# A channel network computed as seven half-sized products, in two phases over three groups of tokens

## What is computed

```python
attn = softmax(mask(q k^T / 8 + slope * -|i - j|)) v      # window of 128 keys, 4 x 8 heads, 576 positions, 64 wide
x = attn as (4, 576, 512)
u = x + ((x^T U) V)^T                                     # U: 576 x 32, V: 32 x 576
y = u + relu(u @ w_ch1) @ w_ch2                           # 512 -> 2048 -> 512: the channel network
h = relu(y @ w_in); a, b = halves of h                    # 512 -> 1024
b = (b - mean(b)) / sqrt(var(b) + 1e-6)
out = (a * (w_spatial @ b + b_spatial)) @ w_out           # 576 x 576 along the positions, then 512 -> 512
```

## Time and profile before

| | us |
|---|---|
| runs: median (lowest to highest) | 774.51 (774.31 to 775.64) |
| profiled execution | 774.84 |
| its span, first to last instruction | 773.1 |
| TensorE busy | 758.4 |
| VectorE / ScalarE / GpSimd busy | 288.1 / 265.2 / 111.3 |
| HBM read / written | 27.83 MB / 4.72 MB |

### The profile page before, as it was taken

One profiled execution on the slowest core, in us unless ns is written; L12 is line 12 of the kernel. 1 busy time (PEld: TensorE's weight loads), 2 busy tenths in 40 slices (PEclk: granted clock), 3 DMA queues, 4 the chain that ended last, 5 costly groups with the idle time before them and its releaser, 6 DMA issues.

```text
span 773.1 us, 12362 instructions
## 1 busy us (share of the span) xinstructions
PE 758.4 (98%) x4584; PEld 647.9 (84%) x4584; DVE 288.1 (37%) x807; ACT 265.2 (34%) x670; POOL 111.3 (14%) x95
## 2 busy tenths in 40 slices
PE   6999999799999999999999999999999999999998
PEld 4777777578888998888888888888899899998998
DVE  6878777531112113111311113111547417435431
ACT  5877777532322112111210102123343243342422
POOL 1212113344451000000000000123410010100100
PEclk9999999999999999999999999999999999999999
DMA  6333331213322000000000000012100010100101
GB/s 170 111 93 122 93 97 60 82 58 106 109 82 69 1 1 1 1 2 0 1 0 0 0 0 0 27 42 74 56 1 1 20 43 0 46 15 0 61 1 62
DMA packets 24692, 33.04 MB, mean 43 GB/s; under 512 B 2768, under 2 KB 11984, under 8 KB 24656
## 3 DMA queue, kind: packets, MB, share of 16 engines
q1 hardware_dynamic: 24656, 32.56, 13.2%
HBM read 27.83 MB, written 4.72 MB: 42 GB/s over the span
## 4 chain that ended last, share of the span: by engine, by line
PE 96%; DVE 1%; issue 1%; DMA 0%; ACT 0%; POOL 0%; SPq 0%; POOLq 0%; DVEq 0%; ACTq 0%
PE bank L1153 9%; PE bank L1154 9%; PE bank L1152 8%; PE bank L1166 6%; PE bank L1167 6%; PE bank L1168 6%; PE bank L1020 4%; PE wide L1035 3%; PE bank L1002 2%; PE bank L1268 2%; PE bank L1270 2%; PE bank L1269 2%; PE bank L1141 2%; PE bank L1139 2%; PE wide L1167 2%; PE wide L1166 2%
## 5 line engine op out<-in xcount | busy, mean ns | idle before, releaser
L834 DVE SCALAR_TENSOR_TENSOR rl<-bank,rh 128x512 fp32r<-128x512 f32 (+1 forms) x80 | 51.0, 638 | 308.3 <-ACT rh L558 308.3
L558 ACT ACTIVATE rh<-bank 128x512 fp32r<-128x512 f32 (+1 forms) x80 | 44.4, 555 | 312.0 <-PE bank L1154 312.0
L1152 PE MATMUL bank<-uh,w1h 128*128 128x512 f32 (+1 forms) x320 | 118.0, 369 | 0.0
L1153 PE MATMUL bank<-uh,w1l 128*128 128x512 f32 (+1 forms) x320 | 117.9, 368 | 0.0
L1154 PE MATMUL bank<-ul,w1h 128*128 128x512 f32 (+1 forms) x320 | 117.9, 368 | 0.0
L1166 PE MATMUL bank<-rh,w2h 128*128 128x512 f32 (+1 forms) x240 | 88.6, 369 | 0.0
L1168 PE MATMUL bank<-rl,w2h 128*128 128x512 f32 (+1 forms) x240 | 88.4, 368 | 0.0
L1167 PE MATMUL bank<-rh,w2l 128*128 128x512 f32 (+1 forms) x240 | 88.4, 368 | 0.0
L467 ACT ACTIVATE sc<-sc,mn 128x256 f32<-128x256 f32 (+1 forms) x144 | 66.9, 468 | 22.0 <-DVE mn L725 22.0
L1152 PEld LDWEIGHTS bank<-uh,w1h 128*128 128x128 f32 x320 | 60.4, 189 | 10.0
L1154 PEld LDWEIGHTS bank<-ul,w1h 128*128 128x128 f32 x320 | 60.4, 189 | 9.9
(11 more groups left out here) (160 smaller groups left out, 1480.4 us busy)
## 6 DMA issues: line engine op xcount, KB each, us to landing
qkraw<-qk SPq DMA_DIRECT2D x32, 288.0 KB, 3.0
out_t<-tok SPq DMA_DIRECT2D x16, 288.0 KB, 2.1
vraw<-v_n SPq DMA_DIRECT2D x16, 256.0 KB, 2.7
w1raw<-w SPq DMA_DIRECT2D x16, 256.0 KB, 2.9
w2raw<-w SPq DMA_DIRECT2D x16, 256.0 KB, 2.6
w1raw<-w_in SPq DMA_DIRECT2D x8, 256.0 KB, 2.8
w1raw<-w_sp SPq DMA_DIRECT2D x4, 288.0 KB, 2.8
w1raw<-w_out SPq DMA_DIRECT2D x4, 256.0 KB, 2.5
```

The costliest lines, as they stand in the source:

```text
L834: dve.scalar_tensor_tensor(out=rl[:, j % 2, 0:width(c)], in0=r_ps[j % 2][:, 0:width(c)], scalar=0.0, in1=rh[:, j % 2, 0:width(c)], op0=ALU ...
L1152: pe.matmul(o, w1h[:, j, k, :], uh[:, k, 0:w], start=(k == 0), stop=False)
L1153: pe.matmul(o, w1l[:, j, k, :], uh[:, k, 0:w], start=False, stop=False)
```

## The change

The product of a 2304 x 512 by a 512 x 2048 matrix, and the one that follows, are both computed with Strassen's scheme in Winograd's form: each operand is cut in 2 x 2 blocks, seven products of half-sized sums replace eight, and the four blocks of the result are sums of the products. The tokens form three groups of 768 (two halves of 384: all channel matmuls have 384 columns).

First phase: 24 units (3 groups x 8 pairs of hidden blocks), each of seven products `up(s, m)` of six matmuls. Some sums of the result are made by letting one product add into the bank of another; for the others ScalarE copies a partial sum out (`keep_p`, after products 1, 6 and 7), and VectorE adds it (`c11`, `c12`, `c22`). ScalarE applies the relu to the sums in place. Each unit's four relu'd blocks (786 KB) are stored to `r_scr` in HBM. The weight sums S1 to S4 are made on VectorE, their high parts on ScalarE, low parts on GpSimd and VectorE: for w1 in the first units, for w2 in units 9 to 14, 17 and 18 (`W2_UNIT`), from where the split w2 goes to `w2_scr` in HBM. `x_sum` (GpSimd) and `x_sum1` (VectorE) make the input sums in place, `hi_xs` and `lo_xs` split them.

Second phase: 168 ring entries (3 groups x 7 products x 8), each of six matmuls in `down(g, m)`. The relu'd blocks come back (`raw` a, b, c, d, over `tok`), GpSimd makes the sums t3, t2, t4 (`r_sum`, two halves of 1536 columns each), VectorE t1 (`r_sum1`); `hi_r` and `lo_r` split one block of 384 columns for each entry into a ring of 5. The split w2 comes back in seven pieces of 2.1 MB (`w2q`). The tensor u was stored to HBM and comes back in `u_in`; GpSimd's `add_res` and VectorE's `dc`, `dc21` add it, and the result goes through HBM (`x2_scr`) to the third stage. That stage's instructions are unchanged; SBUF is laid out anew, its weights come in another order, and its first waits change.

The core of the diff (removed are `up`, `down`, `hi_r`, `lo_r`, `hi_u`, `lo_u`, `keep_x2` and the loads of before):

```diff
+G = 3
+HT = TOK // (2 * G)
+UNITS = NF // 2
+NU = G * UNITS
+RING = 5
+QP = 2 * P
...
+UP = []
+for _s in range(NU):
+    UP += [(_s, 1)] + ([(_s - 1, 4), (_s - 1, 3)] if _s else []) + [(_s, m) for m in (2, 6, 5, 7)]
+UP += [(NU - 1, 4), (NU - 1, 3)]
+UP_AT = {x: n + 1 for n, x in enumerate(UP)}
...
+for _g in range(G):
+    DN += [(_g, 1)] + ([(_g - 1, 3), (_g - 1, 4)] if _g else []) + [(_g, m) for m in (2, 6, 5, 7)]
+DN += [(G - 1, 4), (G - 1, 3)]
+DN_AT = {x: (n + 1) * UNITS for n, x in enumerate(DN)}
+ENTRY = {x: n * UNITS for n, x in enumerate(DN)}
+ENTRIES = [(g, m, kk) for g, m in DN for kk in range(UNITS)]
+W2_UNIT = {9: 0, 10: 1, 11: 2, 12: 3, 13: 4, 14: 5, 17: 6, 18: 7}
...
+LATE = 19
...
+            def load_w1(u):
+                if u >= 2:
+                    sp.wait_ge(w1_low, 2 * (u - 1))
+                    sp.wait_ge(w1_sum, 4 * (u - 1))
+                for i, j in ((0, u), (1, u + UNITS)):
+                    slot = (2 * u + i) % 4
+                    sp.dma_start(w1raw[:, slot, 0:DM], w1[j]).then_inc(w1_in[slot], 16)
+            def store_u(g, r):
+                sp.wait_ge(u_kept, u_ready(g, r))
+                t = slice(2 * g * HT, 2 * (g + 1) * HT)
+                sp.dma_start(u_scr[2 * r:2 * r + 2, :, t].rearrange("k p t -> p k t"),
+                             tok[:, 2 * r:2 * r + 2, t]).then_inc(u_out[r], 16)
+            def store_r(s):
+                g, u = divmod(s, UNITS)
+                sp.wait_ge(r_relu, 3 * (s + 1))
+                sp.wait_ge(c21_done, s + 1)
+                sp.dma_start(r_scr[g, u], r_stage(s)).then_inc(r_out[s % 2], 16)
+            def load_w2(kk):
+                if kk == 0:
+                    sp.wait_ge(w1_low, 2 * UNITS)
+                    sp.wait_ge(w1_sum, 4 * UNITS)
+                else:
+                    sp.wait_ge(w2_low, 2 * kk)
+                    sp.wait_ge(w2_sum, 4 * kk)
+                for i, j in ((0, kk), (1, kk + UNITS)):
+                    sp.dma_start(w1raw[:, i, 0:DM], w2[j * P:(j + 1) * P, :]).then_inc(w1_in[i], 16)
+            def store_w2(kk):
+                sp.wait_ge(w2_slow, kk + 1)
+                sp.wait_ge(w2_low, 2 * (kk + 1))
+                for h, parts in ((0, w2_top), (1, w2_bot)):
+                    sp.dma_start(w2_scr[A11, :, h, kk, :], parts[0]).then_inc(w2_out, 16)
+                    q = parts[1] if h == 0 else parts[1].rearrange("p (q c) -> p q c", c=QP)
+                    sp.dma_start(w2_scr[A12:A22 + 1, :, h, kk, :].rearrange("q p c -> p q c"),
+                                 q).then_inc(w2_out, 16)
+                    sp.dma_start(w2_scr[S1:S4 + 1, :, h, kk, :].rearrange("q p c -> p q c"),
+                                 parts[2]).then_inc(w2_out, 16)
+            def load_w2q(m):
...
+            for s in range(NU):
+                if s + 2 < UNITS:
+                    load_w1(s + 2)
+                if s == 2:
+                    store_u(2, 0)
+                    store_u(2, 1)
+                if s >= 1:
+                    store_r(s - 1)
+                if s in W2_UNIT:
+                    store_w2(W2_UNIT[s])
+                if s + 1 in W2_UNIT:
+                    load_w2(W2_UNIT[s + 1])
+                if s == LATE + 1:
+                    sp.wait_ge(w2_out, 6 * 16 * UNITS)
...
+            sp.wait_ge(up_p, UP_AT[(NU - 2, 3)])
+            load_w2q(5)
+            sp.wait_ge(up_p, UP_AT[(NU - 1, 3)])
+            load_raw(0, "c", 0)
+            load_raw(0, "c", 1)
+            store_r(NU - 1)
+            load_w2q(7)
+            load_w2q(4)
+            sp.wait_ge(u_out[0], 16 * G)
+            sp.wait_ge(u_out[1], 16 * G)
+            sp.wait_ge(c11_done, NU)
+            sp.wait_ge(c12_done, NU)
+            sp.wait_ge(c22_done, NU)
+            load_u(0, 11)
+            load_u(0, 12)
+            for i in range(2):
+                sp.wait_ge(r_out[i], 16 * NU // 2)
+            load_w2q(3)
+            load_u(0, 22)
+            store_x2(0, 11)
...
+            next_raw(1, "a", 1)
...
+            def r_sum(g, m, h):
+                u = slice(4 * h, 4 * h + 4)
+                a, b, c, d = (raw[n][:, u, :] for n in "abcd")
+                if m == 3:
+                    pool.wait_ge(raw_in["b"][h], 16 * (g + 1))
+                    pool.wait_ge(raw_in["c"][h], 16 * (g + 1))
+                    pool.tensor_tensor(b, c, b, ALU.subtract).then_inc(rt3, 1)
+                elif m == 2:
+                    pool.wait_ge(rt3, 2 * g + h + 1)
+                    pool.wait_ge(rk_lo, ENTRY[(g, 1)] + 4 * h + 4)
+                    pool.tensor_tensor(a, a, b, ALU.add).then_inc(rt2, 1)
+                else:
+                    pool.wait_ge(rt2, 2 * g + h + 1)
+                    pool.wait_ge(rk_lo, ENTRY[(g, 2)] + 4 * h + 4)
+                    pool.tensor_tensor(d, d, a, ALU.subtract).then_inc(rt4, 1)
+            def add_res(g, n):
+                kept, done, i = {11: (dp1_kept, dp1_u, 0), 12: (du2_kept, du2_u, 1), 22: (du3_kept, du3_u, 2)}[n]
+                pool.wait_ge(u_back[0 if n in (11, 22) else 1], 32 * g + (16 if n != 22 else 32))
+                for m in range(2):
+                    pool.wait_ge(kept, 2 * g + m + 1)
+                    o = sums_d[:, i, m]
+                    pool.tensor_tensor(o, o, u_in[:, 0 if n in (11, 22) else 1, m], ALU.add).then_inc(done, 1)
...
+            for s in range(NU):
+                g, u = divmod(s, UNITS)
...
+                if s + 2 < UNITS:
+                    w1_low_of(s + 2)
+                if s in W2_UNIT:
+                    w2_low_of(W2_UNIT[s])
+                if u == UNITS - 1 and g < G - 1:
+                    x_sum(g + 1, 4)
+            for g in range(G):
+                add_res(g, 11)
+                for m in (3, 2, 4):
+                    r_sum(g, m, 0)
+                    r_sum(g, m, 1)
+                if g == G - 1:
+                    for m in range(WU):
+                        lo_wc(m)
...
+            def w2_hi_of(kk):
+                act.wait_ge(w2_out, 6 * 16 * kk) if kk else act.wait_ge(xs_lo, 14)
+                for i in range(2):
+                    act.wait_ge(w1_in[i], 16 * (UNITS // 2 + kk + 1))
+                act.activation(w2_top[0].bitcast(F32R), w2_ra[:, 0:QP], ACT.Copy).then_inc(w2_hi, 1)
+                act.activation(w2_top[1].bitcast(F32R), w2_rb.rearrange("p (q c) -> p q c", c=QP),
...
+            def keep_p(s, m):
+                i, kept, freed = {1: (0, p1_kept, c11_done), 6: (1, u2_kept, c12_done),
+                                  7: (2, u3_kept, c22_done)}[m]
+                act.wait_ge(up_p, UP_AT[(s, m)])
+                if s:
+                    act.wait_ge(freed, s)
+                act.activation(sums_u[:, i, :], a_ps[s % 2][:, 0:HT], ACT.Copy).then_inc(kept, 1)
...
+            def hi_r(n):
+                g, m, kk = ENTRIES[n]
+                if n >= RING:
+                    act.wait_ge(rk_used, n - RING + 1)
+                if kk % 4 == 0:
+                    h = kk // 4
+                    if m <= 3:
+                        act.wait_ge(raw_in[RAW_OF[m]][h], 16 * (g + 1))
+                    else:
+                        act.wait_ge({4: rt4, 5: rt1, 6: rt2, 7: rt3}[m], 2 * g + h + 1)
+                act.activation(rk[:, n % RING, 0], raw[RAW_OF[m]][:, kk, :], ACT.Copy).then_inc(rk_hi, 1)
+            def keep_dp(g, m):
...
+            step(B - 1, 2)
+            hi_xs(0, 2)
+            hi_xs(0, 6)
+            step(B - 1, 3)
...
+            for s in range(1, NU):
+                g, u = divmod(s, UNITS)
+                keep_p(s, 1)
+                if u == 0:
+                    hi_xs(g, 7)
+                if s == 1:
+                    hi_t(B - 1)
+                if s + 2 < UNITS:
+                    w1_room(s + 2)
+                    w1_hi_of(s + 2)
+                if s in W2_UNIT:
+                    w2_hi_of(W2_UNIT[s])
+                relu(s - 1, 3)
+                c21(s - 1)
...
+                relu(s - 1, 1)
+                keep_p(s, 6)
...
+                if s + 2 < UNITS:
+                    w1_shi_of(s + 2)
+                if s in W2_UNIT:
+                    w2_shi_of(W2_UNIT[s])
+                relu(s, 0)
+                keep_p(s, 7)
...
+            def room(s):
+                if s >= 2:
+                    dve.wait_ge(r_out[s % 2], 16 * (s // 2))
+            def c11(s):
+                dve.wait_ge(up_p, UP_AT[(s, 2)])
+                dve.wait_ge(p1_kept, s + 1)
+                if s == 0:
+                    dve.wait_ge(xs_lo, 7)
+                    dve.wait_ge(u_out[0], 16)
+                    dve.wait_ge(u_out[1], 16)
+                room(s)
+                dve.tensor_tensor(r_stage(s, 0), e_ps[:, 0:HT], sums_u[:, 0, :], ALU.add).then_inc(c11_done, 1)
...
+            def lo_r(n):
+                g, m, kk = ENTRIES[n]
+                dve.wait_ge(rk_hi, n + 1)
+                dve.tensor_tensor(rk[:, n % RING, 1], raw[RAW_OF[m]][:, kk, :], rk[:, n % RING, 0],
```

(39 more changed lines are left out.)

976 lines of the change are left out of this document (680 added, 296 removed).

## The result

The changed kernel takes 903.2 us (median of 4 runs, 901.4 to 905.7), the kernel before, measured with it, 774.7 (774.3 to 775.6): ratio 1.166, 95% interval 1.164 to 1.168. It is slower by 128 us. The forecast was 890, with a range of 828 to 935. The profiled execution has a span of 903.9 us against 773.1.

What follows compares the result with a forecast made beforehand. The prediction took TensorE's unbroken matmul stream (busy 98% of the span) as the bound. From 774.84 us it took off a 45.2 gain and added 161 of waits: 890.6, stated as 890, range 828 to 935.

Steps and rivals of the forecast that it cites:

- The gain: TensorE's channel matmuls: 395.5 us before, 350.3 us after as 2016 matmuls of 384 columns; 45.2 us saved.
- Rival E: Matmuls of 384 columns come every 0.19 us instead of every 0.174: +32 us; chance 0.02.
- w2 rounds: Units 10 to 14 and 18: chain of stores, load, copies and sums takes 17.2 us against a 7.3 us unit; +58 (48 to 72).
- Rival A: Transfers faster, or loads and stores passing one another: rounds 42, queue 4, first group 28, total 858 us; chance 0.14.
- First group: Start of second phase: GpSimd's add_res waits for u_in, sums stand behind it; +40 us (28 to 48).
- VectorE against GpSimd: Second phase: GpSimd's r_sum steps hold up VectorE's lo_r, both operands in SBUF; +21 us (5 to 34).
- rival B: A long GpSimd step doesn't hold VectorE to its end: 21 falls to 2, first group to 34, total 865; chance 0.11.
- The term of 5: End: hi_wc(8..11) in the middle of the last product and hi_wc(12..16) ahead of relu_v(0); +5 us (1 to 10).
- Start and first units: Start +9 (3 to 14): waits for x sums and lo_xs; first units +12 (5 to 18): longer unit chains, late load_w1(5).
- Queue, group changes, end, clock: DMA queue before second phase +8, first-phase group changes +4, end copies of hi_wc +5, low clock after idle stretches +4 us.
- Rival C: Faster: TensorE isn't held by the w2 rounds, all waits together 42 us, total 771.5 us; chance 0.06.

Runs made afterwards that it cites:

- combined2: Changed kernel with w2 stores in two parts, t3 and t2 on VectorE, t4 of group 0 ahead of add_res, earlier start, c and u_in ahead of w2q(5): 832.6 us.

## Why the prediction was right, and where its terms were off

The forecast is 13 us under the measured 903.2. Two terms were 28 us too small together (groups 1 and 2, and the start with the first units), the third stage 2, and the others some 14 too large together, so part of the closeness is luck: errors of both signs met. The largest terms and their mechanisms held.

**The gain, 45.2 against 46.1.** Right: an entry of six matmuls comes every 1.04 us. Rival E fell: the steps are 0.173 us, though weight loads are listed with 209.

**w2 rounds, 58 against 54.9.** The chain was right link by link, and shown: with its stores divided it loses 22.9. The term was oversized because its data took 8.8 us instead of 9.7. Rival A had the direction right, here and in the queue before the second phase: in the page's two slices from 407 to 452 us, with rows of 16 KB among others, 406 and 416 GB/s were moved, where the forecast had 380, and u_in came at 27.3 instead of 32. It had the size too large both times. The estimate of 7.4 us for a round's data, worked out from the Trainium skill, "DMA: Bandwidth & Descriptors", section "Anatomy of one DMA", which has its fit for another issuing path, is lower than the 8.8 measured with rows of 1 KB. Rival A as a whole, 858, didn't come.

**First group, 40 against 35.8.** Right in mechanism: add_res in GpSimd's order, shown by the run that moves it (14.7 back), and t3 and t2 at 3.4 us each behind it.

**VectorE against GpSimd, 21 against 24.0.** Right, and rival B fell: lo_r stands at 3.82 us beside a step of 3.88, and with the sums cut down group 1 ran without a gap. I had priced it by where the sums stand, 9.5 us at t3 and t2 and 1 at t4, and that is where group 1 lost 9.4 and 1.9. The budget of 62 us in 58.2 says that some 4 us per group stay however the sums are cut; it doesn't give the size.

**The missing term: group 2, 11.0.** The prediction put 5 us on ScalarE's copies of the third stage's weights "in the middle of the last product" and ahead of relu_v. It said nothing of hi_wc(0..7) and hi_x2 among the ring copies of (2, 2) and (2, 4), nor of GpSimd's differences of the same weights beside lo_r, though both stand in the order of the code. The term of 5 itself was too small: 2.5 us of the 11.0 lie in the last product, and the third stage took 7.1 more.

**Start and first units, 21 against 35.2.** The largest error. The stores of u ahead of load_w1(5) were priced as "7.4 us late" within a term of 12, and their move gave back 9.4; units 3 to 7 lost 13.0 in all. Most of the error lies before: the first product came 4.6 us later where the forecast had 2, and from it to unit 3 another 17.6 us were lost, where the forecast had 7 and some 0.9 a unit. The failed step is "half of the first unit behind that: 7": it priced the waits for lo_xs, and neither the w1 sums beside them (5.4 us longer in the trace, though only 2.1 came back when they were moved), nor the waits for ScalarE's copies and VectorE's last tok, nor the slow steps after each wait. How the 17.6 us divide among these isn't settled. The granted clock is 0.91 from 120 to 160 and 0.84 from 160 to 200 us there.

**Queue, group changes, end, clock.** 5.2, 3.9, 7.1 and nothing of its own, against 8, 4, 5 and 4. The clock's share lies in the other terms: up to 0.5 us in a round, and in groups 1 and 2 some 7.8 of the 35.0 us are steps of 0.32 us in place of 0.17, an upper bound, since TensorE would have waited for lo_r in part of that time. Filling the waits raised the mean clock and didn't change the time. At the third stage TensorE waits 4.79 us for ScalarE's vr, which stands behind hi_wc(12..16), as forecast.

**Rival C**, the faster one, didn't come: TensorE was held ahead of product (s, 7) in every round. Other orders didn't reach it either: with all that the runs point to, 823 us remain. By product starts, `combined2` (832.6) still loses some 22 us in rounds, 12 + 5 + 21 in the groups, 19 in units 0 to 7 and 7 in the third stage, and more than the gain of 46 is gone before the rest is counted. I tried no way of making the w2 pieces without the store to memory.

## What to carry to other kernels

A change that takes work from the full engine and gives it to idle ones is worth its gain only if their steps don't form a chain: go through every buffer that is filled, sent away and filled again, and count the time from its last use to its next data against the period in which it is needed. Send each part of such a buffer as soon as it is done, and put nothing that waits for a transfer ahead of work that is ready: these two edits gave back 35 and 12 us here. Where VectorE and GpSimd both take two operands from SBUF, look at what each long step will stand beside, and add their times as if they were one engine for the least that they can cost. Beside a ring of a few entries spread every row of extra copies; that was worth 4 us.

## What the runs showed of the hardware that I had not expected

- The exclusion of VectorE and GpSimd holds both ways and at every length met: 3.82 us listed for a 0.55 us step, 4.95 and 4.86 for 1.76, and GpSimd's 3.4 us step listed with 4.87. The listed start is that of the waiting, so a long listed step isn't slow work. Cutting GpSimd's steps to a quarter left most of the cost of groups 1 and 2 (35.0 us became 28.7, of which 11.0 aren't the sums'), and the two engines then took turns, one lo_r every 1.30 us.
- In unit 11 of the run with filled waits, TensorE ran matmuls 0.17 us apart from 284.5 to 294.8 us, waited 2.8 us, and then ran at steps of 0.32 us, the 1.2 GHz level. In unit 10 a wait of 2.5 us was followed by steps of 0.17.
- With the w2 stores in two parts, the queue moved 292 GB/s at a DMA share of 0.87 from 276 to 320 us, mostly in rows of 1 to 2 KB, and from 430 to 465 us of the changed kernel, with rows of 16 KB among others, 418 at a share of 1.01.
